# Queries and keys of a head turned together, hashed in one product, and placed by copies inside the chip

## The reference

```python
q_bits = (np.einsum('bhsd,dk->bhsk', q, proj) > 0)      # the same for k
mask = q_bucket[:, :, :, None] == k_bucket[:, :, None, :]
scores = np.where(mask, scale * np.matmul(q, k.T), -1000000000.0)
attn = np.exp(scores - scores.max(-1, keepdims=True)); attn /= attn.sum(-1, keepdims=True) + 1e-09
x = attn @ v                                            # (1536, 512): all heads of a row side by side
# then: each row goes to the expert of its largest logit, relu(x @ w1[e]) @ w2[e], times its gate
# then: h = x @ w_in; out = (h * clip(h + 3, 0, 6) / 6) @ w_out
```

## Time and profile before

| | us |
|---|---|
| runs: median (lowest to highest) | 865.62 (865.17 to 866.86) |
| the profiled execution | 865.84 |
| its span, first to last instruction | 864.1 |
| busy in the span: PE, DVE, ACT, POOL | 781.2, 497.5, 382.0, 271.6 |
| chain that ended last, by engine | PE 68%, DVE 15%, issue 8%, ACT 5% |

### The profile page before, as it was taken

How to read it: one execution, slowest core, us unless ns; L and a number is a source line. 1 busy time by engine, 2 the same in 40 slices (tenths; PEclk the granted TensorE clock), 3 DMA queues, 4 the chain that set the end, 5 groups by cost and what they waited for, 6 DMA issues and landing times.

```text
span 864.1 us, 13655 instructions
## 1 busy us (share of the span) xinstructions
PE 781.2 (90%) x4821; PEld 661.0 (76%) x4821; DVE 497.5 (58%) x874; ACT 382.0 (44%) x668; POOL 271.6 (31%) x267
## 2 busy tenths in 40 slices
PE   4899898989898988329999999969999999999998
PEld 2677676767676766229999999949899999989896
DVE  6777878787878886916665555537333231414050
ACT  2455554546464646005555555536333232414150
POOL 5266868686877756520101111000000000000000
PEclk9999999999999999759999999988999999999999
DMA  7030403030414000463555565525010101000000
GB/s 269 28 101 28 101 27 100 27 100 27 111 40 104 9 0 1 159 234 129 207 205 205 225 239 212 213 76 210 13 37 1 49 0 49 0 25 1 25 2 24
DMA packets 36224, 78.09 MB, mean 90 GB/s; under 512 B 3935, under 2 KB 10079, under 8 KB 35680
## 3 DMA queue, kind: packets, MB, share of 16 engines
q1 hardware_dynamic: 32896, 71.33, 24.9%
q0 software_dynamic: 2240, 6.30, 1.9%
q10 hardware_dynamic: 1056, 0.03, 0.1%
HBM read 58.76 MB, written 19.94 MB: 91 GB/s over the span
## 4 chain that ended last, share of the span: by engine, by line
PE 68%; DVE 15%; issue 8%; ACT 5%; DMA 3%; POOL 1%; SPq 0%; DVEq 0%; POOLq 0%; ACTq 0%
PE score_ps L1397 13%; PE score_ps L1398 12%; PE score_ps L1399 12%; PE out_pair L1397 4%; PE out_pair L1398 4%; PE out_pair L1399 4%; DVE rowmax L924 3%; DVE probs_hi L948 2%; PE out_pair L1302 2%; ACT probs L702 2%; PE score_ps L1235 2%; PE prep_ps L1200 2%; PE out_pair L1287 2%; PE out_pair L1288 2%; PE out_pair L1289 2%
## 5 line engine op out<-in xcount | busy, mean ns | idle before, releaser
L586 POOL TENSOR_TENSOR probs_lo<-probs,probs_hi 128x768 fp32r<-128x768 f32 x62 | 117.6, 1917 | 81.4 <-ACT probs_hi L706 81.4
L1397 PE MATMUL score_ps<-w_hi,h_hi 128*128 128x512 f32 x320 | 125.6, 393 | 0.0
L1399 PE MATMUL score_ps<-w_hi,h_lo 128*128 128x512 f32 x320 | 124.6, 389 | 0.0
L1398 PE MATMUL score_ps<-w_lo,h_hi 128*128 128x512 f32 x320 | 124.6, 389 | 0.0
L1156 DVE SCALAR_TENSOR_TENSOR gated<-tclip,score_ps 128x256 f32<-128x256 f32 x48 | 20.2, 421 | 135.4 <-ACT tclip L818 135.1
L1102 DVE TENSOR_TENSOR w_lo<-w_raw,w_hi 128x1024 fp32r<-128x1024 f32 x72 | 85.8, 1222 | 21.4 <-ACT w_hi L716 21.4
L1397 PE MATMUL score_ps<-xT_hi,w_hi 128*128 128x256 f32 x320 | 93.5, 292 | 2.0 <-DVE xT_lo L1149 1.0
L924 DVE TENSOR_REDUCE rowmax<-score_ps 128x1 f32<-128x768 f32 x96 | 89.8, 950 | 6.7 <-PE score_ps L1235 5.7
L1397 PE MATMUL out_pair<-xT_hi,w_hi 128*128 128x256 f32 x320 | 92.5, 289 | 0.0
L1398 PE MATMUL score_ps<-xT_lo,w_hi 128*128 128x256 f32 x320 | 92.2, 288 | 0.0
L1399 PE MATMUL score_ps<-xT_hi,w_lo 128*128 128x256 f32 x320 | 92.0, 288 | 0.0
(11 more groups left out here) (178 smaller groups left out, 1623.8 us busy)
## 6 DMA issues: line engine op xcount, KB each, us to landing
w_raw<-in_moe_w SPq DMA_DIRECT2D x32, 1024.0 KB, 7.0
x_slots<-zrow SPq DMA_DIRECT2D x6, 1026.0 KB, 7.7
rows_in<-x_slots SPq DMA_DIRECT2D x8, 513.0 KB, 8.9
w_raw<-in_moe_w_in SPq DMA_DIRECT2D x4, 1024.0 KB, 5.9
w_raw<-in_moe_w_out SPq DMA_DIRECT2D x4, 1024.0 KB, 12.2
q_raw<-in_q SPq DMA_DIRECT2D x16, 192.0 KB, 3.8
k_raw<-in_k SPq DMA_DIRECT2D x16, 192.0 KB, 3.8
v_raw<-in_v SPq DMA_DIRECT2D x16, 192.0 KB, 2.4
```

The costliest lines, as they stand in the source:

```text
L586: g.tensor_tensor(probs_lo[:, kc, :], probs[:, kc, :], probs_hi[:, kc, :].bitcast(F32), ALU.subtract).then_inc(lo_done_p, 1)
L1397: mm(out_tile, lhs[0], rhs[0], start=first, stop=False)
L1398: mm(out_tile, lhs[0], rhs[1], start=False, stop=False)
L1399: return mm(out_tile, lhs[1], rhs[0], start=False, stop=last)
```

## The change

Queries and keys are loaded side by side into one tile of 128 columns per row group (`qk_raw`), as plain numbers, in pieces of 256 bytes. PE turns both together, unsplit (`turn_qk`). ACT copies the high parts straight from PSUM into `q_ext` (`high_qk`); DVE subtracts that from PSUM for the low parts (`low_qk`). One product hashes both, with a weight tile in which q's and k's rows have columns of their own (`hash_qk`), and one DVE operation writes all bits (`bits`). Since k's parts come out in the lower 64 partitions, under q's, SP moves them with five DMAs per head from SBUF to SBUF (`place_head`). POOL's `split` and DVE's `split_q`, `split_k`, `extend_q` and `extend_k` are gone. At the start the weight loads are issued after head 0's five moves.

```diff
+            def place_head(h, first=False):
+                sp.wait_ge(qk_hi_done, h.i + 1)
+                move(k_ext[h.side][0:D, :], q_ext[h.side][D:2 * D, :]).then_inc(k_hi_placed, 16)
+                move(k_pair[h.side][0:D, :], q_ext[h.side][D:2 * D, :]).then_inc(k_hi_placed, 16)
+                sp.wait_ge(prep_free, lo_use(h, first))
+                move(k_pair[h.side][D:2 * D, :], qk_lo[h.side][D:2 * D, :]).then_inc(k_lo_placed, 16)
+                sp.wait_ge(prep_full, hash_use(h, first))
+                sp.wait_ge(k_lo_placed, h.i * 16 + 16)
+                move(qk_lo[h.side][D:2 * D, :], q_ext[h.side][0:D, :]).then_inc(q_hi_placed, 16)
+                sp.wait_ge(prep_free, hash_use(h, first))
+                move(k_ext[h.side][XR:XR + HB_ROWS, :], q_ext[h.side][XR + HB_ROWS:XR + 2 * HB_ROWS, :]).then_inc(k_bits_placed, 16)
...
+            for side in range(2):
+                load_qk(Head(0, side), first=True)
+                load_v(Head(0, side), first=True)
+            place_head(Head(0, 0), first=True)
             for s in range(LOADS):
                 load_part(0, s, of_expert(0, s), raw_in[s])
+            def next_head(h):
+                load_qk(h.next())
+                place_head(h)
+                load_v(h.next())
...
             def head(h, first=False, second=False, last=False, spare=None):      # POOL
-                if not last and not first:
-                    split(h.next())
                 if spare:
                     spare()
...
+            def low_qk(h):                                                        # DVE
+                dve.wait_ge(qk_hi_done, h.i + 1)
+                v.tensor_tensor(qk_lo[h.side][:, :], prep_ps[:, 0:S], q_ext[h.side][:, :].bitcast(F32),
+                                ALU.subtract).then_inc(prep_free, 1)
+            def bits(h, first=False):
+                dve.wait_ge(prep_full, hash_use(h, first))
+                dve.wait_ge(k_hi_placed, h.i * 32 + 32)
+                v.tensor_scalar(q_ext[h.side][XR:XR + 2 * HB_ROWS, :], prep_ps[0:2 * HB_ROWS, 0:S], above[:, :], weight[:, :],
+                                ALU.is_gt, ALU.mult).then_inc(prep_free, 1)
...
                 take_max(h, 1)
                 if not last:
-                    extend_q(h.next())
+                    low_qk(h.next())
                 take_max(h, 2)
-                if not last:
-                    bits_q(h.next())
                 take_max(h, 3)
                 if not last:
-                    extend_k(h.next())
+                    bits(h.next())
                 take_max(h, 4)
-                if not last:
-                    bits_k(h.next())
                 take_max(h, 5)
...
+            def hash_qk(h, first=False):                                          # PE
+                pe.wait_ge(prep_free, lo_use(h, first))
+                parts = ((proj_hi, q_ext), (proj_lo, q_ext), (proj_hi, qk_lo))
+                for lo, hi in halves:
+                    for n, (weights, tile) in enumerate(parts):
+                        last = mm(prep_ps[0:2 * HB_ROWS, lo:hi], weights[:, :], tile[h.side][:, lo:hi], start=n == 0, stop=n == 2)
+                last.then_inc(prep_full, 1)
...
                 if c == 0:                                                        # PE, max_tile
-                    pe.wait_ge(prep_free, h.i * 5 + 4)
-                    pe.wait_ge(ext_copied, h.i * 2 + 2)
+                    pe.wait_ge(prep_free, h.i * 3 + 2)
+                    pe.wait_ge(k_hi_placed, h.i * 32 + 32)
+                    pe.wait_ge(k_bits_placed, h.i * 16 + 16)
...
                 values(0)
-                prepare(turn_q, second=first)
+                prepare(turn_qk, second=first)
                 values(1)
                 max_tile(h, 2, first)
-                prepare(hash_q)
+                prepare(hash_qk)
                 max_tile(h, 3, first)
                 values(2)
-                prepare(turn_k)
                 max_tile(h, 4, first)
                 values(3)
-                prepare(hash_k)
                 max_tile(h, 5, first)
```

More of the change, by code:

```diff
@@ L64, in hashed_attention_moe_kernel @@
     HB = 4
+    CLEARS = HEADS // 2 - 2
+    assert SLOTS // P % CLEARS == 0 and NT % CLEARS == 0
     assert WC == DC * F2 == FC2 * DM and ST > MT
@@ L338, in max_use, with lo_use, hash_use @@
         def max_use(h, last):
-            return h.i * 5 + (5 if last else 9)
+            return h.i * 3 + (2 if last else 4)
+        def lo_use(h, first=False):
+            return h.i * 3 + (1 if first else 0)
+        def hash_use(h, first=False):
+            return lo_use(h, first) + 1
         LAST = Head((HEADS - 1) // 2, 1)
@@ L600, in head @@
                 sum_v(h, first, second)
-            split(first.next())
             head(first, first=True)
@@ L681, in _, with high_qk @@
             a.activation(scrap[:, 1:2], ident[:, 0:1], ACT.Copy).then_inc(o_copied, 2)
[L683 to L691 removed]
+            def high_qk(h, first=False):
+                act.wait_ge(prep_full, lo_use(h, first))
+                a.activation(q_ext[h.side][:, :], prep_ps[:, 0:S], ACT.Copy).then_inc(qk_hi_done, 1)
             def copy_max(h, last):
@@ L726, in head @@
                     if kc == BY_V and not last:
-                        copy_q(h.next())
-                if not last:
-                    copy_k(h.next())
+                        high_qk(h.next())
                 if spare:
@@ L738, in _ @@
             first = Head(0, 0)
-            copy_turned(q_hl[0], prep_ps, 1)
-            copy_turned(k_lh[0], score_ps[0], 2)
+            high_qk(first, first=True)
             a.activation(back[:, :, 0:D], ident[0:D + 1, 0:D].unsqueeze(1).to_broadcast([D + 1, HEADS, D]), ACT.Copy)
@@ L913, in bits_q @@
-            def bits_q(h):
-                bits(q_ext[h.side], prep_ps, above_q, MASK, h.i * 5 + 2)
-            def extend_k(h):
-                extend(k_ext[h.side], k_lh[h.side][D:2 * D, :], h.i * 5 + 3)
-            def bits_k(h):
-                bits(k_ext[h.side], prep_ps, above_k, -1.0, h.i * 5 + 4)
+                for tile in (proj_hi, proj_lo):
+                    step(v.tensor_copy(tile[:, :], zeros[:, 0:2 * HB_ROWS]))
+                for part in range(2):
+                    rows, col = slice(part * D, part * D + D), part * HB_ROWS
+                    plain = slice(col + part * NBITS, col + part * NBITS + NBITS)
+                    other = slice(col + (1 - part) * NBITS, col + (1 - part) * NBITS + NBITS)
+                    step(v.tensor_copy(proj_hi[rows, plain], proj_sb[rows, :]))
+                    step(v.tensor_tensor(proj_lo[rows, plain], proj_sb[rows, :], proj_hi[rows, plain].bitcast(F32), ALU.subtract))
+                    for tile in (proj_hi, proj_lo):
+                        step(v.tensor_scalar(tile[rows, other], tile[rows, plain].bitcast(F32), -1.0, None, ALU.mult))
@@ L994, in _ @@
             first = Head(0, 0)
-            split_q(first, first=True)
-            split_k(first, first=True)
             projections()
-            extend(q_ext[0], q_hl[0][0:D, :], 1)
-            extend(k_ext[0], k_lh[0][D:2 * D, :], 2)
-            bits(q_ext[0], prep_ps, above_q, MASK, 3)
-            bits(k_ext[0], score_ps[0], above_k, -1.0, 4, uses=2)
+            low_qk(first)
+            dve.wait_ge(setup, setup_bits[0])
+            bits(first, first=True)
             places()
@@ L1206, in hash_bits @@
                 for lo, hi in halves:
-                    mm(ps[0:32, lo:hi], proj_parts[0][:, 0:32], tile[:, lo:hi], start=True, stop=False)
-                    last = mm(ps[0:32, lo:hi], proj_parts[1][:, 0:32], tile[:, lo:hi], start=False, stop=True)
-                last.then_inc(prep_full, uses)
-            def turn_q(h, second=False):
-                if not second:
-                    pe.wait_ge(exp_done, h.i * C - C)
-                turn(q_split, prep_ps, h.i * 2 + 1, h.i * 5)
-            def turn_k(h):
-                turn(k_split, prep_ps, h.i * 2 + 2, h.i * 5 + 2)
```

157 lines of the change are left out of this document (54 added, 103 removed).

## The result

The changed kernel takes 873.92 us (median; 872.43 to 876.70) where the kernel before takes 865.39 (864.48 to 866.86) on the same chip: ratio 1.0091, 95% interval 1.0072 to 1.0110, so it is slower by a little under 1%. The forecast was 841.0 with a range of 835 to 853, so both the sign and the size were wrong. The profiled execution took 876.7 us (span 874.9).

What follows compares the result with a forecast made beforehand. PE was taken as the bound, waiting in even stages for DVE stalled by POOL, otherwise arriving with POOL's chain. From 865.84 us: -22.4, -1.2, -3.9 and +2.6 make -24.9, or 841 us; range 835 to 853.

Steps and rivals of the forecast that it cites:

- Long stages, -22.4 us: Six even stages, 4 to 14, shrink from 22.18 to 18.45 us as POOL's weights piece mostly stops stalling DVE.
- rival 4: Even stages are long for another reason than POOL's meeting DVE, so their gain fails: 863 us, chance 0.05.
- rival 1: In even stages DVE's last subtraction still collides with POOL's first: 12 us of gain lost, 853 us, chance 0.14.
- Odd stages, -1.2 us: Odd stages 5 to 13 take 18.45 us, 0.24 less each, as POOL no longer meets DVE's `extend` casts.
- rival 3: SBUF-to-SBUF moves become the stages' path, losing from 7.8 us per move; at 8.5 us, 888 us; chance 0.05.
- Landing at up to +8.8 costs nothing: A head's first two moves may land 8.8 us into a stage, delaying only row maxima not needed before `cross`.
- Stages 1 and 2, -3.9 us: Stages 1 and 2 take 19.0 us each with one wait less on DVE and POOL; bounds 0 and -5.
- The start, +2.6 us: Before stage 1, the first score tile comes later and head 1's moves queue behind weights; bounds -0.7 and +5.
- The hash's wait: Hash waits for `high_qk` and `low_qk`; PE idles some 0.7 us, covered by less PE work and waiting for POOL.
- rival 2: PE's own work, not POOL's, limits a stage: 17.7 us, 9 us more gain, 832 us, chance 0.08.
- The rule of the Trainium skill: Moves to 64 partitions reach only half the memory's ports: about half a microsecond each, swallowed by slack in the loop.
- the Trainium skill's other rule: New loads in 256-byte pieces, below 512, are written by read and modify: about one microsecond each, swallowed in the loop.

Runs made afterwards that it cites:

- experiment 1: The changed kernel with the clearing issued behind the same head's five moves, ahead of the load of v: 845.71 us, ratio 0.9755.
- Experiment 8: The kernel of experiment 1 with two POOL subtractions, their result unread, put where `split` stood ahead of the weights' piece: 865.09 us, ratio 0.9985.
- experiment 10: The changed kernel with the next head's loads of q and k issued behind the five moves, the clearing in its old place: 844.83 us, ratio 0.9743.
- experiment 2: The changed kernel with 1.0 MB of each clearing in its old place and 0.5 MB one head later: 850.05 us, ratio 0.9785.
- experiment 3: The changed kernel with the first cross product computed five times instead of once in the odd stages: 859.72 us, ratio 0.9908.
- experiment 12: The kernel of experiment 1 with DVE computing the last row maximum three times instead of once in the odd stages: 876.74 us, ratio 1.0112.
- experiment 6: The kernel of experiment 1 with the first expert's four weight loads issued behind head 1's five moves: 841.69 us, ratio 0.9723.
- experiment 9: The kernel of experiment 1 with one of four weight loads behind head 1's moves, three behind head 2's, ScalarE's waits placed to match: 838.47 us, ratio 0.9666.
- experiment 5: The kernel of experiment 1 with PE's hash products behind the fourth score tile instead of ahead of it: 845.39 us, ratio 0.9769.
- experiment 11: The kernel before the change with POOL's piece of the weights put ahead of the two subtractions of `split`: 871.28 us, ratio 1.0056.

## Why the prediction was wrong

*Long stages, -22.4 us: right.* In experiment 1, where nothing disturbs them, the six even stages give 133.17 - 110.61 = -22.6, with 18.44 us each (18.45 forecast). The stalled `v_hi` and the narrow miss of the second collision are in its rows. Experiment 8 puts the collision back and most of the gain is gone, 2.5 of 3.7 us a stage before any fall of the clock, so rival 4 falls; rival 1 falls by the rows of experiment 1. The remaining 1.3 us a stage were right in the sum, but no run shows which part of the change brings them. In the changed kernel they are even shorter, 18.1; I leave open why.

*Odd stages, -1.2 us: the term that failed.* Undisturbed they do it: -1.1 in experiment 1. In the changed kernel they are +32.7. The step was "In the stages behind a clearing they are queued behind it; I find them landing at about +7, inside the same slack." They landed at +9.6 to +11.2. I had taken 7.7 us from the earlier trace rows, the clearing's own landing, as the landing behind a clearing and left out that the change also puts the next head's loads of q and k, 384 KB, between the clearing and the moves; experiment 10 shows that these make the difference. In rival 3 I had named the right mechanism, gave it 0.05, and priced it wrongly: I asked when the move would be the path of every stage (from 7.8 us), not when it would delay one wait of PE.

*"Landing at up to +8.8 costs nothing"* was a fair limit: +8.6 cost no wait of PE and +9.1 did (experiment 2); but nothing was said of what lies beyond it. The price in stage 9 is not the 0.8 us of lateness: it is a wait of 1.45 us and the clock behind it. Experiments 3 and 12 show this half from both sides: with PE kept busy 14 us come back, with PE made to wait 31 us are lost. The earlier trace rows had a window with a clock of 0.92, and I used it as a fact about stages 1 and 2, not as what a wait costs: the old kernel's falls at 52.9 and 73.3 us, of 3.4 us each, come about 2.5 us behind waits of 1.16 and 0.75 us for the negated maximum.

*Stages 1 and 2, -3.9 us:* -5.3, a little past the bound of -5. Both of those waits and both falls are gone, by my estimate 1.9 us and half of 6.8 us.

*The start, +2.6 us: mis-sized.* Measured +6.6 (36.69 to 43.27). The first score tile was forecast at 15.2 and came at 16.66: `bits` ended at 13.8 instead of 13.0, and its own move brought the tile 2.9 us behind that, where I had 2.2. Then head 1: the term that was too small is the landing behind the weights. They were issued at 14.69, not 13.4, the last of them landed at 28.8 (forecast 24), head 2's loads at 31.3 (26), and head 1's second move, for which `bits` waited, at 32.6 (28). The maximum was turned at 36.30 (31.8). From there on nothing was lost, though the clock was at 0.5 until 41.7, since it was at the lower level in the old kernel as well. Experiments 6 and 9 move the weights and have S1 at 35.91 and 36.35, ahead of the old kernel.

*The hash's wait: right*, 0.50 us (0.7 forecast), covered (experiment 5). In that experiment PE waits for POOL's low parts instead, and a stage takes 18.45 us, so rival 2 (17.7) falls.

*The rule of the Trainium skill* (SBUF — State Buffer, "Door 1: The DMA port swizzle"), a transfer to 64 partitions at half of the ports: the moves' packets of 3072 bytes took some 220 ns each, and a loop's three moves together made 203 GB/s (experiment 10, 196.35 to 199.26 us), where the window at the start showed 400 GB/s. The trace agrees. By itself it cost nothing, as said: landings of 2.6 to 3.2 us fit the slack. On the Trainium skill's other rule, of pieces below 512 bytes (DMA: Bandwidth & Descriptors, "Specifications"), the trace settles nothing: the loads of q and k in 256-byte pieces land after 3.0 and 3.4 us with the queue free (experiment 10), 0.6 and 1.0 us later than v in pieces of 1536 bytes. Their packets took 18 ns, those of v 65, so within a packet some 14 GB/s instead of 24; whether that is reading and modifying or a fixed price of each packet was not tried.

## What to carry to other kernels

Before a transfer is put on a queue, list what the same queue carries in the microseconds ahead of it, with the loads that the same edit moves, and compare the last landing with the time at which the first waiter on a shared engine (here DVE, with row maxima behind it) is needed by PE. Price a missed slack by the wait and by the clock that may fall behind it, not by the microseconds of lateness: in this kernel moves that landed 0.3 to 2.4 us past the limit of 8.8 cost 4.5 to 8.7 us a stage. Where a change gives and takes at the same time, a swap of two issues can be worth more than the change: here calling `place_head` ahead of `load_qk` is worth 29 us, by the medians of two chips.

## What the runs showed that I had not expected

- A single wait of PE of 1.2 to 1.5 us was followed by the lower clock for 6.8 to 10.2 us in five odd stages of the changed kernel, though PE was busy again. It does not always follow: one wait of 1.71 us had no fall behind it (experiment 11), and neither had the waits of 1.18 us in the old kernel's even stages. A wait of 0.50 us in every stage brought no fall (experiment 1: clock 1.00 over 270 us). What decides between them was not tried.
- More work on PE made the kernel 14 us faster (experiment 3).
- DVE's stalls coincide with POOL's subtractions of 384 numbers (a cast of 1.38 us in place of 0.55, experiment 11) as they do with the weights' piece of 1024, so taking POOL's work away was worth more than moving it.
- A copy from SBUF to SBUF of 192 KB lands 2.6 to 3.2 us after its issue, near a load of the same size (2.4).
